# VectorE masks one head ahead of its copies in two of five steps, and GpSimd does two operations in an earlier step

## What is computed

```python
scores = scale * q @ k.T                       # 32 heads, 576 x 576 each
thresh = max(scores) - tau                     # by row
attn   = exp(where(scores >= thresh, scores, -1e9) - max); attn /= sum(attn) + 1e-9
x = attn @ v                                   # then x: [4, 576, 512]
u = x + (relu(x.T @ w_tok1) @ w_tok2).T        # token mixing
y = u + relu(u @ w_ch1) @ w_ch2                # channel mixing
h = relu(y @ w_in); c = conv3(h); out = (h * sigmoid(c)) @ w_out
```

## Time and profile before

| | |
|---|---|
| three timed runs | 846.65, 846.94, 847.15 us (median 846.94) |
| profiled execution | 847.35 us, of which the span of instructions is 845.5 us |
| TensorE matmul busy | 823.7 us, 97% of the span |
| VectorE, ScalarE, GpSimd busy | 417.7, 413.3, 257.5 us |
| mean granted clock of TensorE | 0.996 |

### The profile page before, as it was taken

The page is one execution under the profiler, slowest core; times in us unless marked ns, Lnnn a source line. Parts: engine busy times, 40 slices in busy tenths (PEclk is TensorE's granted clock), DMA queues, the critical chain, the costliest instruction groups (busy, mean ns, idle before and its releaser), DMA issues.

```text
span 845.5 us, 15190 instructions
## 1 busy us (share of the span) xinstructions
PE 823.7 (97%) x5656; PEld 670.9 (79%) x5656; DVE 417.7 (49%) x829; ACT 413.3 (49%) x914; POOL 257.5 (30%) x202
## 2 busy tenths in 40 slices
PE   8989999999999998899999999999999999999998
PEld 4657777777777767788888888888899999898996
DVE  6887878878878774401211211211214819155380
ACT  5877888878878884211211211211114727265461
POOL 0251223223323224460200200110391726428170
PEclk9999999999999999999999999999999999999999
DMA  9311111111111204000000000000320010100101
GB/s 267 110 47 48 49 48 47 47 47 47 47 47 49 61 2 150 1 1 0 1 1 1 0 1 1 1 0 1 137 63 2 1 51 1 50 13 0 50 0 62
DMA packets 20906, 32.70 MB, mean 39 GB/s; under 512 B 4416, under 2 KB 11136, under 8 KB 20864
## 3 DMA queue, kind: packets, MB, share of 16 engines
q1 hardware_dynamic: 20864, 32.13, 11.8%
HBM read 27.41 MB, written 4.72 MB: 38 GB/s over the span
## 4 chain that ended last, share of the span: by engine, by line
PE 92%; DVE 3%; ACT 2%; issue 2%; DMA 1%; POOL 0%; ACTq 0%; SPq 0%; DVEq 0%; POOLq 0%
PE score L1238 17%; PE score L1353 12%; PE score L1034 7%; PE out_t L1253 4%; PE turn_y L1253 4%; PE mixed L1253 4%; PE turn_x L1253 4%; PE out_t L1129 4%; PE out_t L1338 4%; PE mixed L1129 4%; PE mixed L1181 3%; PE turn_x L1060 3%; PE turn_y L1338 3%; PE mixed L1338 3%; PE turn_x L1338 3%
## 5 line engine op out<-in xcount | busy, mean ns | idle before, releaser
L956 DVE SCALAR_TENSOR_TENSOR h<-score,h 128x512 fp32r<-128x512 f32 (+1 forms) x60 | 38.3, 638 | 243.5 <-ACT h L726 243.5
L726 ACT ACTIVATE h<-score 128x512 fp32r<-128x512 f32 (+1 forms) x60 | 33.3, 555 | 250.5 <-PE score L1238 250.5
L876 DVE TENSOR_SCALAR_CACHE_REDUCE negs<-score,neg_scale 128x576 f32<-128x576 f32 x144 | 112.7, 816 | 60.1 <-PE score L1034 44.8
L893 DVE SCALAR_TENSOR_TENSOR prob<-negs,thresh,exps 128x576 f32<-128x576 f32 x144 | 129.1, 929 | 0.3 <-ACT thresh L627 0.3
L624 ACT ACTIVATE exps<-negs,neg_max 128x576 f32<-128x576 f32 x144 | 104.7, 772 | 1.9 <-DVE negs L876 1.2
L1034 PE MATMUL score<-qk 64*128 64x288 f32 x512 | 85.6, 435 | 2.6 <-DVE negs L876 2.1
L1238 PE MATMUL score<-uh,w1l 128*128 128x512 f32 (+1 forms) x240 | 86.8, 368 | 0.0
L1238 PE MATMUL score<-uh,w1h 128*128 128x512 f32 (+1 forms) x240 | 86.8, 368 | 0.0
L1238 PE MATMUL score<-ul,w1h 128*128 128x512 f32 (+1 forms) x240 | 86.8, 368 | 0.0
L592 POOL TENSOR_TENSOR zl<-z,zh 128x512 fp32r<-128x512 f32 x32 | 54.2, 1693 | 98.7 <-ACT zh_t L814 98.7
L1034 PEld LDWEIGHTS score<-qk 64*128 64x128 f32 x512 | 47.4, 189 | 28.8 <-issue 13.7
(11 more groups left out here) (184 smaller groups left out, 1968.7 us busy)
## 6 DMA issues: line engine op xcount, KB each, us to landing
qk<-in_qk SPq DMA_DIRECT2D x16, 640.0 KB, 3.9
vm<-in_v SPq DMA_DIRECT2D x16, 320.0 KB, 4.2
result<-ostage SPq DMA_DIRECT2D x16, 256.0 KB, 2.1
w1f<-in_moe_w_ch SPq DMA_DIRECT2D x4, 768.0 KB, 10.8
w2f<-in_moe_w_ch SPq DMA_DIRECT2D x4, 768.0 KB, 7.5
wif<-in_moe_w_in SPq DMA_DIRECT2D x1, 2048.0 KB, 7.9
wof<-in_moe_w_out SPq DMA_DIRECT2D x8, 256.0 KB, 2.6
wt2f<-in_moe_w_tok SPq DMA_DIRECT2D x1, 576.0 KB, 9.4
```

The lines of the kernel that those rows point to most:

```text
L876: nc.vector.tensor_scalar(negs[:, i, h, :].rearrange("p (c s) -> p c s", c=2), raw_of[h], neg_scale[:, 0:1], None, ALU.mult, ALU.min, accu ...
L893: nc.vector.scalar_tensor_tensor(out=prob[:, i, h * S:(h + 1) * S], in0=negs[:, i, h, :], scalar=thresh[:, i, h:h + 1], in1=exps[i][:, h, ...
L956: nc.vector.scalar_tensor_tensor(out=h3[:, n % RING, 1, 0:w], in0=hidden_banks[n % 4][:, 0:w], scalar=0.0, in1=h3[:, n % RING, 0, 0:w].bit ...
```

## The change

In steps 2 and 4 of a body VectorE masks head 0 of unit(s + 1) ahead of its copies, and head 1 behind them as before (with the waits of the mask at head 0). The other steps keep their order. On GpSimd, the wait for the scores of step 1 moves behind `rest_of_token(g - 1, 1)` and `add_u(g - 4)` of step 0's block, so these two run right after the rounding of x in step 0, and only `rest_of_x` waits for step 1's scores. No operation is added or removed. In the diff, `mask(one, (0,))` is the head ahead.

```diff
--- before.py
+++ after.py
@@ -533,11 +533,11 @@
                 if 2 <= k < PAIRS + 2:
                     scores_start(at, 0)
                     round_x(at)
-                    scores_start(at, 1)
                     if even and k >= 4:
                         rest_of_token(g - 1, 1)
                     if not even and 5 <= k < PAIRS:
                         add_u(g - 4)
+                    scores_start(at, 1)
                     rest_of_x(at)
                 if k == PAIRS + 1:
                     add_u(g - 4)
@@ -876,19 +876,20 @@
                     nc.vector.tensor_scalar(negs[:, i, h, :].rearrange("p (c s) -> p c s", c=2), raw_of[h], neg_scale[:, 0:1], None, ALU.mult, ALU.min,
                                             accum_out=neg_max[:, i, h:h + 1]).then_inc(max_done, 1)
 
-            def mask(unit):
+            def mask(unit, heads=(0, 1)):
 
                 g, k, t = unit
                 i = slot_of(k, t)
-                if NT * k + t >= 2:
-                    if t == 1:
-                        dve.wait_ge(t_done, NT * g)
-                    else:
-                        dve.wait_ge(tail_turned, FULL * g + max(t - 1, 0))
-                if t == 0 and k >= 1:
-                    dve.wait_ge(sum_done, g)
-                dve.wait_ge(thr_done, NT * g + t + 1)
-                for h in range(2 if t < FULL else 1):
+                if 0 in heads:
+                    if NT * k + t >= 2:
+                        if t == 1:
+                            dve.wait_ge(t_done, NT * g)
+                        else:
+                            dve.wait_ge(tail_turned, FULL * g + max(t - 1, 0))
+                    if t == 0 and k >= 1:
+                        dve.wait_ge(sum_done, g)
+                    dve.wait_ge(thr_done, NT * g + t + 1)
+                for h in heads if t < FULL else (0,):
                     dve.wait_ge(exp_done, tiles_to(g, t) + h + 1)
                     nc.vector.scalar_tensor_tensor(out=prob[:, i, h * S:(h + 1) * S], in0=negs[:, i, h, :],
                                                    scalar=thresh[:, i, h:h + 1], in1=exps[i][:, h, :],
@@ -934,12 +935,15 @@
             def body(at):
                 for s in range(NT):
                     two, one = at.unit(s + 2), at.unit(s + 1)
+                    ahead = one and s in (2, 4)
+                    if ahead:
+                        mask(one, (0,))
                     if two:
                         copy_out(two)
                     if s == 4 and at.units:
                         invert_sums(at)
                     if one:
-                        mask(one)
+                        mask(one, (1,) if ahead else (0, 1))
                     if s == 1 and at.k == PAIRS:
                         split_first_u()
                     if s == 3 and at.pv:
```

## The result

| | before | after |
|---|---|---|
| median of the timed runs | 846.94 us | 851.16 us |
| lowest to highest | 846.57 to 847.15 | 849.27 to 852.53 |
| profiled execution, its span | 847.35, 845.5 | 852.43, 850.6 |
| mean granted clock, profiled execution | 0.996 | 0.992 |

The ratio is 1.0045, with a 95% interval of 1.0033 to 1.0056: 0.45% slower. The time of the kernel after goes with its clock: at a mean of 0.995 it took 849.27 and 849.39 us, at 0.994 851.11 and 851.21, at 0.992 and 0.991 852.43 and 852.53.

What follows compares the result with a forecast made beforehand. The prediction took TensorE, with its clock, to bound the kernel. Its terms, pair 0 +1.4, clock +3.2, pair 1 0, pair 2 -2.0, steady pairs 0, summed to +2.6 on the 846.94 us median: 849.5, range 845.2 to 853.0.

Steps and rivals of the forecast that it cites:

- The sum of +2.6: Whole kernel: all terms added, 1.4 + 3.2 + 0 - 2.0 + 0 us, with one fall of the clock, chance 0.38.
- What bounds the kernel, and the steady pairs at 0: TensorE bounds; in pairs 4 to 15 the mask's 0.23 us stall goes, but ScalarE's short tile still delays the tail: 0.
- GpSimd's reorder at 0: Pairs 4 to 15: the moved addition holds a step 0 mask, the subtraction one mask instead of two; 0 us.
- Pair 0, +1.4: Masks ahead wait for thresholds in steps 2 and 4, delaying copies and the next pair's scores; +1.4 us, bounds +0.8 to +1.7.
- The clock in pair 1, +3.2: A 1.8 us TensorE pause before pair 1's first scores halves the clock for 6.8 us; +3.2 us, bounds 0 and 3.4.
- Pair 1, 0: Step 3's copies start 0.5 us earlier, step 4's 0.6 later, transposes as now; 0 us, bounds -0.6 to +0.5.
- Pair 2, -2.0: Tile 3's masks end earlier, transposes start 1.2 us sooner, the clock doesn't fall there; -2.0 us, bounds -1.0 to -2.5.
- The sign that I named: In pair 2, tile 3's masks would end before 59.2 us in the profile.
- the first (no fall): Rival: the clock stays up in pair 1; -0.6 us, 846.3 us, no change; chance 0.30.
- The second (faster): Rival: pair 0 loses 0.8, pair 2 gains 2.5, odd pairs keep 0.1 to 0.2 each; 844.6 us; chance 0.14.
- The third (a second fall in step 4 of pair 1): Rival: the clock falls again where TensorE's 0.49 us pause grows by 0.6; +5.8 us, 852.7 us; chance 0.14.
- The fourth: Rival: the reorder does nothing, tiles being held as before; 847 us; chance 0.04.

Runs made afterwards that it cites:

- without the early step 4: The kernel after, with head 0's mask ahead dropped in body 0 and in step 4 of bodies 1 to 3; 845.50 us, ratio 0.9977.
- both runs with the pause filled: Two matmuls with unread results put ahead of pair 1's first scores: on the kernel after 850.34 us, on the kernel before with body 0's masks ahead 850.51.
- body 0 only: The kernel before, with VectorE's mask ahead only in body 0, steps 2 and 4; 851.86 us, ratio 1.0046; with two added TensorE matmuls 850.51.

## Why the prediction was right, and where its sizes were off

The forecast was 849.5 us in a range of 845.2 to 853.0; it came to 851.16, slower, by the mechanism named. The sum of +2.6 holds for an execution without further falls, which comes to +2.3; in part that is luck, since two errors of 0.7 and 0.8 us inside pair 2 cancelled. Two more falls of the clock, which the sum didn't hold, made the rest. Step by step:

- **What bounds the kernel, and the steady pairs at 0: right.** Two steady pairs take 39.42 us, the short tile ends at 201.68 and the tail's transpose starts behind it. The run with the head ahead from pair 4 on (ratio 0.9994) and that without the early step 4 show it by time. That ScalarE's short tile was the second wait is shown by the runs that moved it.
- **GpSimd's reorder at 0: right.** In the kernel after, one mask is held in step 0 of pair 9 (1.39 us from 191.06, where 0.81 is usual) and none behind the subtraction, where one took 2.08.
- **Pair 0, +1.4: right.** 1.5 us, read from both runs with the pause filled. Tile 4's copy came at 20.98 (forecast 20.9), tile 1's at 27.25 (27.0).
- **The clock in pair 1, +3.2: right in kind, too large by 0.5.** The fall lay from 27.7 to 34.5, where 29 to 37 was named, and cost 2.67 us against the same kernel with the pause filled.
- **Pair 1, 0: right.** From pair 1 to 2 the kernel after takes 18.50 us instead of 18.64. The mark of body 2 is 5.02 us late, more than the 4.19 of pair 0 and the fall together, because TensorE's wait for step 4's copies grew from 0.49 to 1.63 us; a step later that is made good, as I had argued.

Here the Trainium skill had spoken against the forecast: "TensorE: Matmul & The Clock Gate", its table of rules for authors, warns only of idle gaps longer than these. The runs don't agree with it: falls came in, or within 0.7 us behind, pauses of 0.71, 1.62, 1.66 and 1.86 us, and with the pause filled the clock stayed up. But such a pause doesn't make a fall each time: 0.71 us in the kernel before, 1.63 in pair 1 of the kernel after and 1.44 in pair 2 with VectorE's part alone were followed by none.

- **Pair 2, -2.0: near, by two errors that cancelled.** VectorE's part alone, whose clock stayed up there, gains 20.82 - 19.08 = 1.74. Step 2's mask gives 1.1 (I had 1.2). The missing fall gives 1.4, where I had 0.6 to 0.8, because I took the rest of the slow stretch for VectorE's time; the run with step 2 of body 0 alone shows 1.4 with VectorE's work unchanged. The head ahead in step 4 takes 0.8 to 0.9 back, which I had put at nothing. The sign that I named, tile 3's masks ending before 59.2, was put in the time of the kernel before: they end at 63.16, which is 4.4 us after tile 4's scores start, where it was 5.6 before and 4.5 in the forecast.
- **What the sum left out: two further falls.** One came at 68.7, behind a pause of 1.43 us for the copies of pair 2's step 4, where the mask ahead stands before the copies as in pairs 0 and 1. From pair 2 to 3 TensorE takes 20.47 us with it and 19.08 in the profile of VectorE's part alone, which lacks it: 1.4. I had worked out step 4 for pairs 0 and 1 and not for pair 2. The other came in body 15 and cost 1.30 (19.42 us against 18.12).

The ledger of the profiled execution: pair 0 +1.5, the fall at 27.7 +2.7, pair 1 -0.1, pair 2 -1.7, the fall at 68.7 +1.4, body 15 +1.3: +5.1. VectorE's part alone, whose profile has only the first fall, checks it: the first four terms are +2.4, its marks give +2.3, and it took 849.62. The two runs of the kernel after with the highest clock took about as much, 849.27 and 849.39. The forecast was the time of an execution with one fall, and the typical one, at 851.16, lies above the 848.6 to 850.6 that I had given to one fall. The stated range held it because its upper end stood for two falls, the second of them in another place. That the slower timed runs have more falls is read from their mean clock only; where these lie isn't seen.

Of the rivals, the first (no fall) is what the run with body 0 only and the pause filled shows at body 2. The second (faster) failed as argued, at ScalarE's short tile. The third (a second fall in step 4 of pair 1) didn't come in the profile of the kernel after, but did once its first pause was filled. It was the right kind of rival, tied to too few places. The fourth fell with pair 2.

## What to carry to other kernels

Before removing a wait of the bounding engine, look at its next instruction: if that one waits for another engine that ends just as late, the first wait will only change its name; move both, and each begins to count (0, 0.49 and 0.78 us a pair here). An operation put ahead of another in a fixed order brings its own wait along, and where a pipeline is still filling, as in pairs 0 to 2, that wait stands before everything; make such a reorder start where the queues are full. The two steps differ, too: in pair 2 the head ahead gave 1.1 us in step 2 and cost 0.9 in step 4. Price a pause of TensorE in a sparse stretch by what the clock may cost behind it (1.0 to 2.7 us a fall here), not by its length alone.

## What was not expected of the hardware

- The clock fell in different places in executions of the same instructions. In body 15 it fell in four profiles (the kernel after, step 2 of body 0 alone, step 2 of bodies 1 and 2, the change without its early step 4) and stayed up in the others, that of the kernel before among them. It cost 1.30 us in the first and 1.50 in the third. Two of the four have no change of code within 200 us of it. What decides it isn't settled.
- Every fall seen lasted some 3.4 or 6.8 us, at 0.50. By the table those of 6.8 us cost 2.7 us ahead of pair 1's tile 4 and 1.4 and 1.9 behind the wait of 1.32 us in pair 2; those of 3.4 us cost 1.05 behind that wait, 1.4 to 1.6 elsewhere in pairs 1 and 2, and 1.3 and 1.5 in body 15.
- The same pause wasn't always followed by the same fall. At or behind the wait of 1.32 us in pair 2 the clock fell for 6.8 us in the kernel before, for 3.4 in two profiles with the same code up to there, and not at all with step 2 of body 0 alone or with ScalarE's order changed on the kernel before. An earlier fall doesn't settle it: with one of 3.4 us there was none near 60, but with step 4 of body 0 alone, and with body 0 only, a fall of 6.8 us came first and another of 3.4 behind that wait. With the first pause of the kernel after filled, the clock fell 20 us later, after a pause that it had stood before. The profiles are too few to show a rule.
- The same instructions' time varies with it: the kernel with step 4 of body 0 alone took 849.26 us at a mean clock of 0.995 and 853.47 at 0.990.
